# Softmax's maximum as a bias of eight exponentials per head instead of a subtraction over the tile

## What is computed

```
scores = scale * q @ pooled_k.T            # (B, H, 576, 72)
scores = scores - max(scores, axis=-1)
attn = exp(scores); attn = attn / (sum(attn) + 1e-9)
x = attn @ pooled_v                        # 2304 tokens x 512
logits = x @ w_gate + log1p(exp(x @ w_noise)) * noise   # two largest experts a token
x = sum over 2 picks of weight * relu(x @ w1[e]) @ w2[e]
h = x @ w_in; out = max(0.01 * h, h) @ w_out
```

## Time and profile before

| | us |
|---|---|
| median of three executions | 1104.15 |
| lowest and highest of them | 1102.9, 1104.63 |
| the profiled execution, its own time | 1103.91 |
| its span in the trace | 1102.2 |
| TensorE busy | 1033.5 |
| VectorE busy | 378.9 |
| ScalarE busy | 272.5 |
| mean granted TensorE clock | 0.967 |

### The profile page before, as it was taken

The page is one execution under the profiler, slowest core; times in us unless marked ns, Lnnn a source line. Parts: engine busy times, 40 slices in busy tenths (PEclk is TensorE's granted clock), DMA queues, the critical chain, the costliest instruction groups (busy, mean ns, idle before and its releaser), DMA issues.

```text
span 1102.2 us, 16369 instructions
## 1 busy us (share of the span) xinstructions
PE 1033.5 (94%) x5180; PEld 870.6 (79%) x5181; DVE 378.9 (34%) x678; ACT 272.5 (25%) x497; POOL 379.6 (34%) x413
## 2 busy tenths in 40 slices
PE   5988289999999999999999995899999999999998
PEld 4887268888888888888888884788888888888887
DVE  5988542122212221222122212653333333333222
ACT  3443012222222222222222220232222222222222
POOL 3338691280917355371908202950100100000000
PEclk9988589999999999999999997899999999999999
DMA  8945452151524333251514212421101101001000
GB/s 296 337 145 189 178 160 77 57 180 39 171 67 140 97 111 127 80 158 49 173 63 144 95 38 72 147 78 39 39 20 58 39 20 58 20 1 39 1 1 38
DMA packets 53779, 105.75 MB, mean 96 GB/s; under 512 B 7408, under 2 KB 7536, under 8 KB 53744
## 3 DMA queue, kind: packets, MB, share of 16 engines
q1 hardware_dynamic: 35312, 63.33, 18.1%
q10 hardware_dynamic: 12672, 23.07, 6.3%
q0 software_dynamic: 5760, 18.88, 5.1%
HBM read 77.47 MB, written 27.79 MB: 95 GB/s over the span
## 4 chain that ended last, share of the span: by engine, by line
PE 79%; issue 9%; DVE 7%; POOL 3%; DMA 1%; ACT 1%; SPq 0%; POOLq 0%; DVEq 0%; ACTq 0%
PE ps L603 23%; PE ps L605 23%; PE ps L604 23%; PE ps L629 3%; POOL w_split L467 2%; PE ps L561 2%; PE ps L610 1%; PE ps L539 1%; POOL w_split L465 1%; PE ps L671 1%; DVE maxima L906 1%; PE ps L549 1%; DVE x L1149 1%; DVE k_sum L892 1%; DMA k_raw<-in_kT_dram 1%
## 5 line engine op out<-in xcount | busy, mean ns | idle before, releaser
L467 POOL TENSOR_TENSOR w_split<-w_raw,w_split 128x512 fp32r<-128x512 f32 x144 | 186.3, 1294 | 12.0
L465 POOL TENSOR_SCALAR w_split<-w_raw 128x512 fp32r<-128x512 f32 x144 | 92.3, 641 | 226.7 <-PE ps L605 224.7
L603 PE MATMUL ps<-w_split,xs_hi 128*128 (+1 forms) x344 | 138.4, 402 | 3.9 <-DVE xs_lo L1108 3.9
L603 PE MATMUL ps<-w_split,hT_hi 128*128 (+1 forms) x344 | 139.0, 404 | 2.0 <-DVE hT_lo L1115 2.0
L605 PE MATMUL ps<-w_split,hT_lo 128*128 (+1 forms) x344 | 135.4, 394 | 0.0
L605 PE MATMUL ps<-w_split,xs_lo 128*128 (+1 forms) x344 | 134.7, 391 | 0.0
L604 PE MATMUL ps<-w_split,hT_hi 128*128 (+1 forms) x344 | 134.6, 391 | 0.0
L604 PE MATMUL ps<-w_split,xs_hi 128*128 (+1 forms) x344 | 134.6, 391 | 0.0
L492 POOL DMA_INDIRECT y_in<-y_blocks,y_rows x36 | 34.8, 968 | 269.1 <-DVE x L1149 194.8
L603 PE MATMUL ps<-x_hi,w_split 128*128 128x512 f32 (+1 forms) x320 | 120.5, 377 | 1.4 <-DVE x_lo L1157 1.4
L604 PE MATMUL ps<-x_lo,w_split 128*128 128x512 f32 (+1 forms) x320 | 118.8, 371 | 0.0
(11 more groups left out here) (147 smaller groups left out, 1505.3 us busy)
## 6 DMA issues: line engine op xcount, KB each, us to landing
w_raw<-in_wall_dram SPq DMA_DIRECT2D x160, 256.0 KB
xs<-x_sorted ACTq DMA_DIRECT2D x45, 256.0 KB, 2.7
y_blocks<-y_sb ACTq DMA_DIRECT2D x43, 256.0 KB, 2.0
k_raw<-in_kT_dram SPq DMA_DIRECT2D x16, 288.0 KB, 5.5
q_sb<-in_qT_dram SPq DMA_DIRECT2D x18, 256.0 KB, 5.2
v_raw<-in_vT_dram SPq DMA_DIRECT2D x16, 288.0 KB, 5.2
out_dram<-h_sb SPq DMA_DIRECT2D x10, 256.0 KB, 2.0
x_sorted<-zero_rows SPq DMA_DIRECT2D x9, 256.0 KB, 4.1
```

The costliest lines, as they stand in the source:

```text
L465: pool.tensor_scalar(hi, w_raw[:, a, :], 1.0, 0.0, ALU.mult, ALU.add).then_inc(split_hi, 1)
L467: pool.tensor_tensor(lo, w_raw[:, a, :], hi.bitcast(F32), ALU.subtract).then_inc(split, 1)
L603: pe.matmul(out_ap, lhs_hi, rhs_hi, start=first, stop=False)
```

## The change

The subtraction on VectorE goes. VectorE multiplies the 128x8 maxima by minus the scale in place, and ScalarE computes, for each of the eight heads, exp(scale * score + bias) with that head's column as bias, reading 72 columns from PSUM and writing them to `probs`. So `centred` now says that the bias is ready, and not that the score banks have been read; TensorE's score waits for `exped` in its place. The wait for the transposes that last read the same half of `probs` moves from VectorE to ScalarE. The order of all other instructions on all engines stays.

```diff
@@ score(t), TensorE
                 if t >= 1:
-                    pe.wait_ge(centred, t)
+                    pe.wait_ge(exped, t)
@@ exp_probs(t), ScalarE
                 act.wait_ge(centred, t + 1)
-                pr = probs[:, t % 2, :, :].rearrange("p h k -> p (h k)")
-                act.activation(pr, pr, ACT.Exp, scale=SCORE_SCALE).then_inc(exped, 1)
+                if t >= 2:
+                    act.wait_ge(probs_turned, t - 1)
+                for h in range(HEADS):
+                    ins = act.activation(probs[:, t % 2, h, :], scores[:, h // 4, h % 4, :], ACT.Exp,
+                                         bias=maxima[:, h:h + 1], scale=SCORE_SCALE)
+                ins.then_inc(exped, 1)
@@ centre(t), VectorE
                 dve.wait_ge(maxed, t + 1)
-                if t >= 2:
-                    dve.wait_ge(probs_turned, t - 1)
-                dve.tensor_tensor(probs[:, t % 2, :, :].rearrange("p (a b) k -> p a b k", a=2), scores,
-                                  maxima[:, :].rearrange("p (a b) -> p a b", a=2).unsqueeze(3)
-                                  .to_broadcast([P, 2, HEADS // 2, KEYS]),
-                                  ALU.subtract).then_inc(centred, 1)
+                dve.tensor_scalar(maxima[:, :], maxima[:, :], -SCORE_SCALE, None, ALU.mult).then_inc(centred, 1)
```

## The result

| | before, us | changed, us | ratio, 95% interval |
|---|---|---|---|
| first set of runs | 1104.39 | 1122.57 | 1.0174 (1.0142 to 1.0206) |
| second set, beside three experiments | 1104.37 | 1117.09 | 1.0116 (1.0087 to 1.0145) |

The changed kernel is slower in both sets. The forecast was 1122, range 1109 to 1133. The four executions of the first set lie between 1121.3 and 1128.2 us and those of the second between 1116.8 and 1118.4, while the kernel before has the same median in both; so the kernel before does not show this spread.

The account below looks back on a forecast made before the run. It took the 18-tile loop to set the first xs load, with TensorE's own expert work after it. On 1103.91 us, +12.5 at full clock and +5.4 for the clock gave +18, 1122 us, range 1109 to 1133.

Parts of the forecast that it names:

- The path: Up to the first xs load at 136.04 us: a microsecond longer in the 18-tile loop is one on the span.
- The ring: Loop: score waits for the previous tile's exponentials, behind transposes and copy; 5.2 us a tile at full clock.
- The price of an exponential: ScalarE, eight exponentials of 72 columns with bias: 0.267 us each start to start, 2.14 us for eight.
- Rival (c): ScalarE's queue: exponentials pipeline at 0.12 us each and the kernel is faster, -5, 1099 us; chance 0.06.
- nine plain spacings: Loop: nine score-to-score spacings under 5.2 us, 38.4 us together, become 48.0 at full clock: +9.6.
- The seven others: Loop: remaining score spacings, 45.2 us, set by VectorE's routing, TensorE's ranks and clock; together -0.2 us.
- The tail: After the last score: the last exponentials cost 1.46 us more, +1.5.
- The two big terms: Before the first xs load: +12.5 us at full clock, and +5.4 for three more loop tiles at 1.2 GHz.
- Rival (a): Loop: the clock falls no oftener, so only +12.5 us, 1116 us; chance 0.16.
- Rival (b): Loop: clock low in half of it, eight more spacings, +27 us, 1131 us; chance 0.11.
- (d): ScalarE in the loop: its 45 idle us of 84 take up the work, +0, 1104 us; chance 0.04.
- Rival (e): ScalarE: the bias makes each exponential dearer than 0.30, at 0.36 us, 1134 us; chance 0.06.

Follow-up runs that it names:

- 3: Changed kernel with one maximum over all eight heads of a token and one exponential over 2 x 288 columns instead of eight: 1102.72 us (0.9987).
- 8: Changed kernel with the bias left out of the eight exponentials: 1102.39 us (0.9985).
- 2: Changed kernel with the exponentials put ahead of the previous tile's copy in ScalarE's queue: 1111.76 us (1.0063).
- 11: Changed kernel with sixteen exponentials of 36 columns, each head in two halves with the same bias, instead of eight of 72: 1149.87 us (1.0417).
- 7: Kernel before, with the score waiting for exped instead of centred and one exponential as before: 1105.52 us (1.0006).
- 6: Kernel before, with the in-place exponential split into eight of 72 columns without bias, subtraction kept: 1106.55 us (1.0022).
- experiment 4: Changed kernel with eight transposes of the identity into an unused part of a bank behind each tile's attend: 1110.2 us (1.0052).

## Why the prediction came out

**The path.** Right: all of the difference lies before the first load of xs (+19.2 us, from 136.04 to 155.26), and what follows is 964.5 instead of 966.2 us (967.7 in the second set's trace).

**The ring.** Right, and shown from both sides: a shorter group of exponentials in the same ring (3, 8) takes the loss away, the copy out of the ring (2) takes a part of it, and a longer group (11) lengthens the ring by just what it is longer. The wait without the long group (7) and a longer group without the wait (6) cost 1.4 and 2.5 us in the medians. Predicted 5.2 us, measured 5.12. But that is two errors that nearly cancel. The eight exponentials took 1.80, not 2.14, and what lies between took 0.3 more: the score was counted as 1.02 and is 1.06, the transposes as 0.87 and the copy waits for all of their 1.04, and from the last exponential to the score it is 0.14, where I had counted 0.15 for all four hand-offs.

**The price of an exponential.** 0.267 from L753 in the earlier trace rows was the wrong row, although it had the same number of columns. Eight of 72 columns take 0.154 start to start in place in SBUF ((1.33 - 0.249) / 7), 0.112 from PSUM and 0.210 from PSUM with a bias. My lower bound of 0.12, from the two L823 and from 320 and 1024 columns, was right for the instruction without its bias. What decided was the 0.10 of the bias, which no row of before showed. Rival (c) put the turning point at 0.18 an exponential: 0.112 gave 1102.39 and 0.210 gave 1117 to 1123, so it lies between. Why L753 stands 0.267 apart is open.

**Full clock, loop.** The kernel with TensorE kept busy is the nearest to a changed kernel at full clock. Its nine plain spacings are 48.3 us, predicted 48.0: +9.9, predicted +9.6. The seven others are 43.3, predicted 45.0: -1.9, predicted -0.2. Tile 1's score came 1.3 later after tile 0's, predicted 1.6.

**The tail.** Wrong: +1.5 predicted, -0.8 in the changed kernel's first trace, -2.7 in its second and -2.0 in experiment 4 (36.4 us from tile 17's score to the load, before 38.4). The last two attends before ran at 1.2 GHz, in 3.55 and 3.68 us, and the ranks of the third turn stand behind them. In the changed kernel's first trace one of the two did (1.91 and 3.68); in its second none, and with TensorE kept busy none. In order of time: tiles 16 and 17 before, the same in the second trace of the changed kernel and its load of xs (35.65 us after tile 17's score at 112.03), then tiles 15 to 17 of experiment 4:

```profile
104.36 3.55 PE L561 MATMUL ps<-v_pool,probsT 72*128 72x82 f32 x16
109.58 3.68 PE L561 MATMUL ps<-v_pool,probsT 72*128 72x82 f32 x16 [1.68 <-DVE gate_prod L928]
```
```profile
117.80 1.91 PE L561 MATMUL ps<-v_pool,probsT 72*128 72x82 f32 x16
121.60 1.98 PE L561 MATMUL ps<-v_pool,probsT 72*128 72x82 f32 x16 [1.89 <-DVE gate_prod L927]
...
147.68 2.55 DMA xs<-x_sorted
```
```profile
107.87 1.91 PE L561 MATMUL ps<-v_pool,probsT 72*128 72x82 f32 x16
111.72 1.91 PE L561 MATMUL ps<-v_pool,probsT 72*128 72x82 f32 x16
115.51 1.98 PE L561 MATMUL ps<-v_pool,probsT 72*128 72x82 f32 x16 [1.00 <-DVE gate_prod L930]
```

I had added the exponentials to a tail that was held by attends at low clock, and did not ask which. The lengths nearly give it: 1.1 for the exponentials, less 1.6 and 1.7 for the two attends, makes -2.2, near the -2.7 of the second trace.

**The two big terms.** What was mis-sized is the split: +12.5 for the change at full clock and +5.4 for the clock. By experiment 4 the first is +5.8 us in the medians and +7.3 in the traces (9.9 - 1.9 + 1.3 - 2.0). Of the 5.2 us between 7.3 and 12.5, 3.5 are the tail and 1.7 the seven other spacings; the ring's own +9.6 was right. The rest goes with the clock: 18.2 - 5.8 = 12.4 us in the first set of runs, 12.7 - 5.8 = 6.9 in the second. In the loops of the traces it is 10.9 and 5.2. The low stretches were nine and five, where I had counted six, the three of before and three more. So the sum of 18 is right to the microsecond in one set and 5 us too high in the other, and where it was right that was luck: a first term twice too large and a clock term half as large as it should be. This split is an estimate and not shown to the microsecond, since the kernel before has low stretches of its own and the added transposes cost 4 us there.

Rival (a), that the clock falls no oftener, is false: 0.85 and 0.91 in the loop against 0.94. Its +12.5, 1116, happens to lie at the second set's 1117, by another mechanism. Rival (b), eight more low tiles, is near the first set's count of six more, but not its time: its sum, with the same 12.5 in it, was 1131. Rivals (c) and (d) fell with the bias. Rival (e), 0.36 an exponential, is false: 0.21. The busy time of ScalarE rose by 19 us (20 to 30 predicted), VectorE's fell by 9.7 (10 predicted).

How many tiles fall into low stretches is not settled by the program alone. The two sets differ by 5 us with the same instructions; what decides between them was not tried, and stays open.

## What to carry to other kernels

Before an operation is split and moved to an engine that looks idle, ask who reads a single buffer last: if the split operation becomes the last reader, its whole length goes into a ring with everything that stands ahead of it in its queue, and an engine that is idle for over half of the time buys nothing. Price a group of small instructions in the form that it will have, operands included: here the same eight cost 1.03 us and no time without a bias per partition, and 1.80 us and 13 to 18 us a run with one. When a ring leaves TensorE a rest in every round, add what its clock will lose, and look for one large instruction (here a maximum shared by the heads) or for another order in the queue.

## What the runs showed of the hardware

- A [128,1] bias costs an ACTIVATE from PSUM 0.10 us start to start and 0.08 in length; 36 columns instead of 72 save 0.031 of 0.210 us (0.179 start to start, from 3.01 us for sixteen of 322 ns), so by an estimate from these two lengths some 0.15 of it does not depend on the columns.
- ScalarE's exponentials of 72 columns from PSUM to SBUF run closer together (0.112 us) than in place in SBUF (0.154), in groups of eight with no wait in them. Whether the memory or the writing in place makes the difference was not tried.
- Matmuls that serve nothing saved 6.9 us in the changed kernel: loop clock 0.91 to 0.98, TensorE's rest 1.27 to 0.41 us a tile. Where TensorE itself was the bound they cost 4 us.
- The granted clock in the loop of one and the same program was 0.85 in one profiled execution and 0.91 in another.
